# Attention scores one unit further ahead, and the unit before the tile, in the first steps of a fused attention and two-stage MLP kernel

## The reference

```
scores = 0.125 * q @ k^T, masked to 0 <= i - j < 64
x = softmax(scores) @ v                       # to 1152 tokens x 512
h = x @ w_in                                  # 512 -> 2048
g = max(h, 0) + log1p(exp(-abs(h)))
y = g @ w_out                                 # 2048 -> 512
p = domain_probs / (sum + 1e-9)
out = sum over e of p[:, e] * (max(y @ w1[e], 0) @ w2[e])
```

## Time and profile before

| | us |
|---|---|
| median of 3 runs | 659.83 (659.53 to 660.18) |
| profiled execution | 660.2 |
| its span | 658.1 |
| TensorE busy | 645.2 (98%) |
| VectorE busy | 290.4 (44%) |
| ScalarE busy | 232.4 (35%) |
| GpSimd busy | 88.9 (14%) |

### The profile page before, as it was taken

The page is one execution under the profiler, slowest core; times in us unless marked ns, Lnnn a source line. Parts: engine busy times, 40 slices in busy tenths (PEclk is TensorE's granted clock), DMA queues, the critical chain, the costliest instruction groups (busy, mean ns, idle before and its releaser), DMA issues.

```text
span 658.1 us, 9966 instructions
## 1 busy us (share of the span) xinstructions
PE 645.2 (98%) x3688; PEld 600.2 (91%) x3688; DVE 290.4 (44%) x708; ACT 232.4 (35%) x584; POOL 88.9 (14%) x85
## 2 busy tenths in 40 slices
PE   7979999999999999999999999999999999999998
PEld 6778999999999999989898989898989898989896
DVE  5877665577646585612252512252512251512121
ACT  5777665566444564401040402040402040402020
POOL 1343333323333333000000000000000000000000
PEclk9999999999999999999999999999999999999999
DMA  8903330123000030300030400030300030110101
GB/s 327 349 30 134 123 129 1 33 97 128 1 1 1 0 128 33 98 0 1 0 127 1 129 0 1 0 127 0 127 0 0 0 127 0 64 48 0 48 0 48
DMA packets 11569, 40.56 MB, mean 62 GB/s; under 512 B 2320, under 2 KB 2320, under 8 KB 10256
## 3 DMA queue, kind: packets, MB, share of 16 engines
q1 hardware_dynamic: 11536, 40.13, 17.0%
HBM read 37.77 MB, written 2.36 MB: 61 GB/s over the span
## 4 chain that ended last, share of the span: by engine, by line
PE 93%; DVE 2%; DMA 2%; ACT 1%; issue 1%; POOL 1%; SPq 0%; DVEq 0%; ACTq 0%
PE ps L718 25%; PE ps L753 20%; PE ps_pT L718 10%; PE ps_score L718 10%; PE ps_score L753 10%; PE ps L738 8%; PE ps_score L738 4%; PE ps_o L738 4%; DMA unit_in<-in_units 2%; PE ps_score L679 1%; PE ps_pT L705 1%; ACT prob L351 1%; DVE prob L480 1%; PE ps_pT L692 1%; POOL sp_c L306 1%
## 5 line engine op out<-in xcount | busy, mean ns | idle before, releaser
L718 PE MATMUL ps<-xy_hi,wa_hi 128*128 128x384 f32 (+1 forms) x320 | 109.1, 341 | 0.7 <-issue 0.7
L440 ACT ACTIVATE hid_hi<-ps 128x384 fp32r<-128x384 f32 x48 | 23.6, 492 | 241.7 <-PE ps L718 241.6
L718 PE MATMUL ps<-xy_hi,wa_lo 128*128 128x384 f32 (+1 forms) x320 | 107.3, 335 | 0.0
L718 PE MATMUL ps<-xy_lo,wa_hi 128*128 128x384 f32 (+1 forms) x320 | 107.2, 335 | 0.0
L306 POOL TENSOR_TENSOR sp_c<-sp_e,sp_c 128x384 f32<-128x384 f32 x48 | 64.7, 1348 | 141.4 <-DVE sp_c L510 141.4
L753 PE MATMUL ps<-wb_hi,hid_lo 128*128 128x512 f32 x192 | 74.9, 390 | 0.0
L753 PE MATMUL ps<-wb_lo,hid_hi 128*128 128x512 f32 x192 | 74.9, 390 | 0.0
L753 PE MATMUL ps<-wb_hi,hid_hi 128*128 128x512 f32 x192 | 74.7, 389 | 0.0
L658 DVE SCALAR_TENSOR_TENSOR part<-ps,gate,part 128x512 f32<-128x512 f32 x24 | 18.0, 751 | 104.8 <-PE ps L753 104.8
L718 PEld LDWEIGHTS ps<-xy_hi,wa_hi 128*128 128x128 f32 x320 | 60.1, 188 | 2.2 <-issue 0.8
L718 PEld LDWEIGHTS ps<-xy_lo,wa_hi 128*128 128x128 f32 x320 | 60.1, 188 | 0.4
(11 more groups left out here) (115 smaller groups left out, 1245.8 us busy)
## 6 DMA issues: line engine op xcount, KB each, us to landing
unit_in<-in_units SPq DMA_DIRECT2D x8, 1024.0 KB, 6.7
raw_a<-in_w SPq DMA_DIRECT2D x16, 512.0 KB, 4.2
raw_b<-in_w SPq DMA_DIRECT2D x16, 512.0 KB, 3.9
raw_a<-in_w_in SPq DMA_DIRECT2D x8, 512.0 KB, 5.3
raw_b<-in_w_out SPq DMA_DIRECT2D x8, 512.0 KB, 4.5
out_dram<-part SPq DMA_DIRECT2D x9, 256.0 KB, 2.0
part<-in_units SPq DMA_DIRECT2D x2, 1024.0 KB, 13.6
unit_in<-in_units SPq DMA_DIRECT2D x2, 384.0 KB, 7.7
```

What stands on the lines that cost most here:

```text
L440: act.activation(hid[0][:, f, :], up_banks[f % 4][:, 0:CH], ACT.Relu).then_inc(h_hi, 1)
L718: m = pe.matmul(bank[:, 0:CH], wa[a][:, f, k, :], xy[x][:, bass.ds(c, 1), k, :], start=(k == 0 and i == 0), stop=(k == KT - 1 and i == 2))
```

## The change

On TensorE, the scores of unit 10 come before the last products that start tile 1's up projection, and in steps 0 and 1 the scores of units 11 and 12 follow the tile's up projection (before, the scores of units 10, 11 and 12 preceded the up projections of steps 0, 1 and 2). On VectorE, unit 10 is masked ahead of the inverse of unit 9, and units 11 and 12 between the low part and the maximum of tiles 0 and 1; `split_down(0, 0)` follows the normalisation of unit 9. On ScalarE, the exponentials of a unit precede the absolute value of the tile in steps 0 to 2. On GpSimd, the normalisation of a unit precedes `lost` of the tile in steps 0 to 2, and the third of the later low halves waits for unit 8 instead of unit 9.

```diff
@@ GpSimd
-            for i in range(len(FIRST_SPLIT), 2 * len(FIRST_SPLIT)):
-                pool.wait_ge(norm_done, min(i + 4, SCORED))
+            for i, unit in zip(range(len(FIRST_SPLIT), 2 * len(FIRST_SPLIT)), (7, 8, 8, 9)):
+                pool.wait_ge(norm_done, unit + 1)
                 up_low_half(i // 2, i % 2)
             for k in range(STEPS):
+                if k < LAG:
+                    normalise(k + SCORED)
                 lost(k // FT, k % FT)
-                if k + SCORED < N_UNITS:
+                if LAG <= k < N_UNITS - SCORED:
                     normalise(k + SCORED)
@@ ScalarE
                 if k < LAG:
                     copy_pT(k + WEIGHED)
-                absolute(n, f)
                 if k < LAG:
                     softmax_exp(k + SCORED)
-                elif k < N_UNITS - WEIGHED:
+                absolute(n, f)
+                if LAG <= k < N_UNITS - WEIGHED:
                     copy_pT(k + WEIGHED)
@@ VectorE
                 if j == SCORED - 1:
                     down_high(0)
-                    split_down(0, 0)
+                    masked_scores(SCORED)
                 row_inverse(j)
                 normalise_first(j)
+                if j == SCORED - 1:
+                    split_down(0, 0)
...
-                if k + SCORED < N_UNITS:
+                if LAG <= k < N_UNITS - SCORED:
                     masked_scores(k + SCORED)
                 if k < LAG:
                     row_inverse(k + SCORED)
                     rounded(n, f)
                     if k > 0:
                         hidden_low((k - 1) // FT, (k - 1) % FT)
+                    if k < LAG - 1:
+                        masked_scores(k + SCORED + 1)
                     relu_ln(n, f)
@@ TensorE
             weigh_values(UPC - 1)
+            scores(SCORED)
             start_up(1, 0)
...
                 if s < LAG:
                     transpose_probs(s + WEIGHED)
-                    scores(s + SCORED)
...
-                if LAG <= s < N_UNITS - SCORED:
+                if s < LAG - 1:
+                    scores(s + SCORED + 1)
+                elif LAG <= s < N_UNITS - SCORED:
                     scores(s + SCORED)
```

## The result

The changed kernel takes 655.71 us (655.06 to 657.37, 5 runs) against 659.84 (5 runs): ratio 0.9940, 95% interval 0.9926 to 0.9955. That is 4.1 us faster; 3.65 had been forecast, to 656.2 us.

A forecast was written before the change was run, and what follows sets the result against it. Before 51.45 us TensorE waits for a loop of ScalarE, VectorE and GpSimd, afterwards its own work bounds. Gains 2.40 + 1.34 - 0.09 = 3.65 us from 659.83 give 656.2 us; own range 655.6 to 657.2, full range 655.0 to 657.6.

The forecast's parts named there:

- The block behind 51.45 us slides: TensorE from the second tile's first down product on: its own work, unchanged, moving as one block with that product's start.
- Entry: Start of the stretch up to unit 11's exponentials: unit 10 at 29.37, unit 11 at 33.11 instead of 35.51, gain 2.40 us.
- The turn from unit 11 to 12: One turn of the loop over ScalarE, VectorE and GpSimd, exponentials to exponentials: 4.08 us against 5.42, gain 1.34.
- To unit 13: Turn from unit 12 to 13, mask again behind the addition and a split: 6.12 us against 6.03, 0.09 lost.
- From there to down(0,1): From unit 13 to the second tile's first down product: order as before, so that product comes 3.65 us earlier, at 47.80.
- Sum: Gain at unit 13 from the entry and two turns: 2.40 + 1.34 - 0.09 = 3.65 us.
- rival 1: VectorE's rounding isn't held by GpSimd's normalisation: entry gain 2.9, total gain 4.65, 655.2 us; chance 0.15.
- The new one on the maximum of tile 1: TensorE's tile 3 waits for a bank freed by VectorE's maximum of tile 1: about 0.4 us, covered by the 1.1.
- The 0.5 us for a copy: The unit's copy ahead of tile 3's bank wait holds TensorE some 0.5 us more, under the same cover.
- Rival 2: Unit 12's scores on TensorE wait for their inputs' transfer: gain only 1.15, 658.7 us; chance 0.07.
- Rival 3: Tile's chain becomes the bound, at VectorE's maximum and GpSimd's subtraction: slower, 0.84 us a step, 662.3 us; chance 0.03.
- Rival 4: ScalarE gets to unit 10 no sooner, so the change doesn't do what it says; chance 0.05 with all else.

The follow-up runs named there:

- b2: Changed kernel with VectorE's cast of the first down weight moved behind the normalisation of unit 9, just ahead of `split_down(0, 0)`: 655.73 us.
- a1: Changed kernel with ScalarE's order undone: in steps 0 to 2 the tile's absolute value first, the unit's exponentials second: 656.21 us.
- a4: Changed kernel, but in steps 0 to 2 GpSimd's normalisation also waits until the rounding of that step's tile is done: 656.02 us.
- the second profile: The changed kernel itself, unaltered, timed and profiled once more beside later runs: 655.69 us.
- a3: Kernel before with only the unit-first orders on ScalarE and GpSimd in steps 0 to 2; scores and masks not moved: 659.75 us.
- b1: Changed kernel with the next unit's mask between row inverse and rounding in steps 0 to 2, unit 13 scored and masked in step 2: 654.76 us.
- b3: b1 with VectorE's cast of the first down weight also moved behind the normalisation of unit 9: 654.41 us.
- a6: Changed kernel with the split of the first down weight and GpSimd's third later low half put back as before: 655.73 us.

## Why the prediction was right

**The block behind 51.45 us slides.** Right: from down(0,1) to the end of the span there are 606.65 us before and 606.78 after.

**Entry.** Unit 10's exponentials were reckoned 3.16 us behind the values of unit 7 (29.37 - 26.21), measured 3.24 and 3.23. Unit 11's were reckoned at 6.90, with the rounding of tile 0 held; measured 6.47 where it was not held, 7.06 where it was. The step was right as a mechanism and blind to one thing: the cast of the down weight waits for its transfer in both profiles, which it didn't at 27.46 in the rows, so unit 10's normalisation comes 5.63 and 5.35 us behind the values of unit 7, not 5.06 (31.27 - 26.21). That puts it within 0.2 us of tile 0's rounding, and which goes first changes from execution to execution. That is 0.4 us of stretch. The larger spread of the changed kernel (655.06 to 657.37, against 659.53 to 660.18 before) is not explained by it. Of its ten executions the three longest (656.15, 656.24 and 657.37) are the three with a mean granted clock of 0.997, where the others have 0.999 or 1.000. And b2, whose profile has the rounding held, spreads as widely (655.22 to 657.29), with 0.997 in its two longest. In the profiles of a1, a4 and b2, which have 0.997 too, the granted clock was 0.50 (1.2 GHz) from 10 to 12 us, behind 2 us in which TensorE was busy for 0.62 to 0.90. That lies ahead of everything the change touches. No profile was taken of those three executions of the changed kernel, so that it was the same there is not shown.

**The turn from unit 11 to 12.** Reckoned 4.08, measured 4.13 and 3.94, against 5.42. How near the first comes is in part luck. VectorE goes on 0.13 us behind the end of the normalisation (34.59 to 34.72), not the 0.27 reckoned; but the row sum came 1.50 us behind the exponentials, not 1.30, as it stood behind the late addition of tile 0. In the second profile the row sum takes its 1.30 and VectorE goes on after 0.14 (35.28 to 35.42), which makes nearly all of the difference to 4.08. **To unit 13**: reckoned 6.12, measured 6.00 both times. **From there to down(0,1)**: 4.49 us before and after, as assumed.

**Sum.** Reckoned stretch 47.80 - 26.21 = 21.59 us, measured 21.09 and 21.49. The gain of 4.1 us against 3.65 is inside the forecast's own range. The term that was mis-sized is the entry: 2.40 reckoned, 2.83 and 2.24 measured in the two profiles. The 2.83 is what rival 1 gave for an entry without the hold (2.9). The median of 655.71 us lies halfway between the forecast's 656.2 and rival 1's 655.2, so the time doesn't tell the two apart; the durations of the roundings do.

**TensorE's waits.** The new one on the maximum of tile 1 was forecast as 0.4 and is 0.35 (0.23 in the second profile); it is covered, as reckoned, by the last one, which was 1.1 and is 0.65 and 0.68. The 0.5 us for a copy shows in the second profile alone (0.46; the profile names no releaser there, but ScalarE's copy had ended 0.10 us before).

**The rivals.** Rival 1, no hold, is refuted for tiles 1 and 2 by 0.77 and 0.57, and by a4; for tile 0 the rounding went unheld in one of two profiles, because it started first, not because there is no hold. Rival 2: TensorE waits for no transfer there. Rival 3: the wait on the maximum is 0.35 us and covered. Rival 4: unit 10 started where reckoned.

## What to carry to other kernels

When several engines go round one loop for every unit of work, and the busiest engine waits for its product, add up a turn from start to start: what shortens it is to take work off the loop (here the mask, which needed nothing of the turn it stood in), more than to reorder the work that stays on it. VectorE and GpSimd working on SBUF side by side hold each other (additions of 1.17 us for 0.55, normalisations of 1.21 for 0.83): an order that frees one pair may just collide in another (a3), and making one wait for the other moves the cost to whoever is next in GpSimd's queue (a4). Stop once the busiest engine's list of waits is empty (b1); a move on another engine then bought nothing (b3).

## What the runs showed that was not expected

One kernel, two executions: two operations of VectorE and GpSimd that start within 0.2 us of each other came in one order and then in the other, and with it went 0.61 us of rounding (0.35 against 0.96). It was no toss-up in these two profiles: the rounding hung on TensorE and ScalarE, which had started 0.3 us earlier in the first, and the normalisation on a transfer that ended the cast's wait at 27.24 in both. The time that an operation is held shows in the profile as its own duration, not as idle time ahead of it, on both engines (a normalisation of 0.83 us took 1.21 in a4). And a row sum of only three elements a partition waits for GpSimd's whole operation as well, yet gets in between two of them that stand back to back (0.44 us in a6).
